# Gated linear attention ahead of two dense layers: units of 128 tokens computed as two halves of 64

## What is computed

```python
f = 1.0 / (1.0 + np.exp(-f_logit))
for t in range(S):
    state = f[:, :, t, :, None] * state + np.einsum('bhd,bhe->bhde', k[:, :, t], v[:, :, t])
    y[:, :, t] = np.einsum('bhd,bhde->bhe', q[:, :, t], state)
x = y.transpose(0, 2, 1, 3).reshape(B * S, H * D)
h = x @ w_in                                   # first block
x = (np.maximum(h, 0) + np.log1p(np.exp(-np.abs(h)))) @ w_out
h = x @ w2_in                                  # second block
out = np.where(h >= 1, h, np.where(h <= -1, 0, (h + 1) ** 2 / 4)) @ w2_out
```

## Time and profile before

| | |
|---|---|
| median of 3 runs | 919.57 us (918.11 to 922.22) |
| the profiled execution: its own time, and its span | 920.22 us, 918.3 us |
| TensorE matmul, weight load | 898.0 us (98%), 742.0 us (81%) |
| VectorE, ScalarE, GpSimd | 512.9 us, 446.4 us, 67.3 us |
| granted TensorE clock over the span | 0.998 of 2.4 GHz |

### The profile page before, as it was taken

One profiled execution on the slowest core, in us unless ns is written; L12 is line 12 of the kernel. 1 busy time (PEld: TensorE's weight loads), 2 busy tenths in 40 slices (PEclk: granted clock), 3 DMA queues, 4 the chain that ended last, 5 costly groups with the idle time before them and its releaser, 6 DMA issues.

```text
span 918.3 us, 14986 instructions
## 1 busy us (share of the span) xinstructions
PE 898.0 (98%) x5810; PEld 742.0 (81%) x5810; DVE 512.9 (56%) x875; ACT 446.4 (49%) x839; POOL 67.3 (7%) x59
## 2 busy tenths in 40 slices
PE   7889999999999999999999999999999999999996
PEld 4789988888888888888888888888888888888884
DVE  5976765566555555654355655555555555555453
ACT  5876665565565555665577533232332332333222
POOL 2112211111111111110000100000000000000000
PEclk9999999999999999999999999999999999999999
DMA  8622222112111311400033200200200200200001
GB/s 276 208 80 65 84 70 74 43 42 77 43 42 54 96 55 42 149 33 1 23 116 98 75 1 1 69 1 1 70 1 0 69 1 1 70 1 10 25 1 37
DMA packets 22300, 50.57 MB, mean 55 GB/s; under 512 B 2384, under 2 KB 3152, under 8 KB 22224
## 3 DMA queue, kind: packets, MB, share of 16 engines
q1 hardware_dynamic: 22224, 49.55, 17.2%
HBM read 40.11 MB, written 9.44 MB: 54 GB/s over the span
## 4 chain that ended last, share of the span: by engine, by line
PE 92%; DVE 2%; ACT 2%; issue 1%; DMA 1%; POOL 1%; SPq 0%; DVEq 0%
PE h_ps L458 15%; PE h_ps L460 14%; PE h_ps L459 14%; PE y_ps L458 14%; PE y_ps L460 14%; PE y_ps L459 14%; PE a_ps L514 2%; PE c_ps L528 1%; PE a_ps L557 1%; PE c_ps L540 1%; PE c_ps L547 1%; PE c_ps L532 1%; PE c_ps L502 1%; DMA qkf_sb<-qkf 1%; POOL qkf_sb L433 1%
## 5 line engine op out<-in xcount | busy, mean ns | idle before, releaser
L818 DVE TENSOR_TENSOR g_lo<-gate,g_hi 128x512 fp32r<-128x512 f32 (+1 forms) x208 | 135.2, 650 | 355.3 <-ACT g_hi L664 354.4
L458 PE MATMUL h_ps<-x_hi,w_hi 128*128 128x512 f32 (+1 forms) x624 | 237.9, 381 | 4.4 <-issue 2.1
L458 PE MATMUL y_ps<-g_hi,w_hi 128*128 128x512 f32 (+1 forms) x624 | 233.4, 374 | 3.5 <-DVE g_lo L818 3.5
L459 PE MATMUL h_ps<-x_lo,w_hi 128*128 128x512 f32 (+1 forms) x624 | 232.8, 373 | 0.0
L460 PE MATMUL h_ps<-x_hi,w_lo 128*128 128x512 f32 (+1 forms) x624 | 232.7, 373 | 0.0
L460 PE MATMUL y_ps<-g_hi,w_lo 128*128 128x512 f32 (+1 forms) x624 | 232.6, 373 | 0.0
L459 PE MATMUL y_ps<-g_lo,w_hi 128*128 128x512 f32 (+1 forms) x624 | 232.5, 373 | 0.0
L652 ACT ACTIVATE soft<-h_ps 128x512 f32<-128x512 f32 x96 | 57.4, 598 | 266.1 <-PE h_ps L460 265.0
L648 ACT ACTIVATE soft<-h_ps 128x512 f32<-128x512 f32 (+1 forms) x112 | 60.0, 536 | 169.7 <-PE h_ps L460 169.7
L458 PEld LDWEIGHTS h_ps<-x_hi,w_hi 128*128 128x128 f32 x624 | 117.3, 188 | 29.4 <-issue 4.7
L458 PEld LDWEIGHTS y_ps<-g_hi,w_hi 128*128 128x128 f32 x624 | 117.4, 188 | 25.9 <-DVE g_lo L818 5.3
(11 more groups left out here) (76 smaller groups left out, 619.1 us busy)
## 6 DMA issues: line engine op xcount, KB each, us to landing
w_raw<-w SPq DMA_DIRECT2D x32, 384.0 KB, 6.0
qkf_sb<-qkf SPq DMA_DIRECT2D x24, 448.0 KB, 4.5
v_sb<-v SPq DMA_DIRECT2D x24, 256.0 KB, 4.5
qkf_sb<-qkf SPq DMA_DIRECT2D x24, 224.0 KB, 3.0
qkf_sb<-x_mid SPq DMA_DIRECT2D x6, 768.0 KB, 5.5
out<-y_sb SPq DMA_DIRECT2D x18, 256.0 KB, 2.2
x_mid<-y_sb SPq DMA_DIRECT2D x15, 256.0 KB, 2.3
x_mid<-y_sb SPq DMA_DIRECT2D x6, 128.0 KB, 1.9
```

The source lines that it names most:

```text
L458: nc.tensor.matmul(out_ap, hi1, hi2, start=start, stop=False, skip_group_check=True)
L459: nc.tensor.matmul(out_ap, hi1, lo2, start=False, stop=False, skip_group_check=True)
L818: nc.vector.tensor_tensor(g_lo[:, t % 2, 0:g.n], gate[:, t % 2, 0:g.n], g_hi[:, t % 2, 0:g.n].bitcast(F32), ALU.subtract).then_inc(glo_don ...
```

## The change

Units of 4 and later are computed as two halves of 64 tokens. Scores are then taken only within a half (four blocks of 64 by 64 for each pair of heads, on four quarters of the array), and half 1 gets what half 0 added through an extra state `mid`. The result of half 0 goes to bank `c_ps`, that of half 1 to `b_ps`. In `result` the part from scores uses row tile 0 for half 0 and row tile 1 for half 1. The part from states puts the even heads on row tile 0 and the odd ones on row tile 1, first each into the bank that its row tile has used so far and then, after a wait of TensorE for its own matmuls (`own_done`), into the other bank. `increment` of a unit moves behind `turn_keys` and in front of `score` of the next unit, and `result` of a unit comes one slot after that. The main slots of units 4 to 23 are 4 slots of the program earlier in full groups, those of units 4 to 8 all fall into the second group of two (slots 1, 4, 7, 10 and 12 of it), and stages of an empty unit 24 end the chain.

```diff
-MAIN = {2: (7, 12), 3: (3, 7, 11), 4: (0, 4, 8, 12)}
+HALVES = (0, 1, 1, 2, 3)
+HALVES_FAST = (0, 1, 1, 2, 3)
+FAST_STEPS = (1, 4, 7, 10, 12)
...
+def make_steps():
+    out = {2: 7, 3: 12}
+    for u in range(B, UNITS + 1):
+        out[u] = FT + FAST_STEPS[u - B] if u <= 2 * B else 2 * FT + 4 * (u - 2 * B - 1)
...
SP:
                         if u < UNITS:
+                            sp.wait_ge(e_done, u - RING + 1)
+                            load_f(u)
                             unit_left(u - RING)
-                            load_unit(u)
+                            load_qk(u)
+                            load_v(u)
...
GpSimd:
+            pool.memset(state[:], 0.0).then_inc(consts, 1)
+            pool.memset(mid[:], 0.0).then_inc(consts, 1)
...
TensorE:
+            def increment(u):
+                pe.wait_ge(k_tok_done, u + 1)
+                ...
+                for p in range(PAIRS):
+                    for a in range(2):
+                        for half, bank in ((0, a_ps), (1, b_ps)) if has_future(u) else ((0, a_ps),):
+                            t = slice(half * T2, (half + 1) * T2)
+                            mm = nc.tensor.matmul(bank[64 * a:64 * a + D, 5 * T2 + p * D:5 * T2 + (p + 1) * D],
+                                                  k_tok[t, p, 64 * a:64 * a + D], vu[t, 2 * p + a, data_columns(a)], ...)
+            def score(u):
+                pe.wait_ge(q_done, u + 1)
+                for p in range(PAIRS):
+                    for half in range(2):
+                        for a, bank in ((0, a_ps), (64, b_ps)):
+                            mm = nc.tensor.matmul(bank[t, (p + 1) * T2:(p + 2) * T2], k[a:a + D, p, t], q[a:a + D, p, t], ...)
+            def result(u):
+                pe.wait_ge(masked, masks_until(min(u + 1, UNITS - 1)))
+                pe.wait_ge(k_tok_done, min(u + 2, UNITS))
+                pe.wait_ge(total_done, states_until(u) - B)
+                for a in range(2):
+                    for k, columns in ((2 * a, main_columns(a)), (1, rest_columns(a))):
+                        for j in range(PAIRS):
+                            for half, t in enumerate(tokens):
+                                nc.tensor.matmul(result_ps(half, k)[HALF * j:HALF * (j + 1), :], vu[t, 2 * j + a, columns],
+                                                 sc[t, a, j, :], ...)
+                pe.wait_ge(state_done, u - B + 1)
+                pe.wait_ge(mid_done, u - B + 1)
+                for other in range(2):
+                    for main in (True, False):
+                        for j in range(PAIRS):
+                            for a in range(2):
+                                half = a ^ other
+                                ... mm = nc.tensor.matmul(result_ps(half, ...), st[rows, first:first + HALF], q[rows, j, tokens[half]], ...)
+                    if other == 0:
+                        mm.then_inc(own_done, 1)
+                        pe.wait_ge(own_done, u - B + 1)
...
+                    if s == 0:
+                        pe.wait_ge(xlo_done, max(u - 1, B))
+                        turn_keys(u); increment(u - 1); score(u)
+                    if s == 2:
+                        result(u - 1)
...
VectorE (mask at stage 1 of unit u, middle(u - 1) behind it; the state at stage 4):
+            def mask(u):                      # one instruction for both banks, 128x1024
+            def middle(u):
+                nc.vector.tensor_tensor(block(mid), increment_ps(a_ps), block(state[:, batch(u)]), ALU.add)
+                nc.vector.tensor_tensor(total[0:ROWS], increment_ps(b_ps), block(mid), ALU.add)
+        # stage 4: state = total * by, by = a 112x4 copy made in prep_end
```

More of the change, by code:

```diff
@@ L166, in build @@
         k_tok = sb("k_tok", [P, PAIRS, ROWS])
-        state = sb("state", [P, B, PAIRS, HEAD])
+        state = sb("state", [P, B, PAIRS * HEAD + REST])
+        mid = sb("mid", [P, PAIRS * HEAD + REST])
+        total = sb("total", [P, PAIRS, D])
+        by = sb("by", [P, B, PAIRS])
         causal = sb("causal", [P, P])
+        causal2 = sb("causal2", [P, T2])
         ident = sb("ident", [P, P])
@@ L272, in same_banks_before, with place, half_scores, block @@
             return 0 if u == 2 else u - 1
+        def place(u):
+            g = [g for g in LAYER0 if g.unit <= u][-1]
+            return g, slice((u - g.unit) * P, (u - g.unit + 1) * P)
+        def half_scores(u):
+            return scores[:, u % 2].rearrange("p b t -> p (b t)").rearrange("p (a b t) -> p a b t", a=2, b=PAIRS)
+        def block(t):
+            return t[0:ROWS, 0:PAIRS * HEAD].rearrange("p (q e) -> p q e", q=PAIRS)[:, :, REST:HEAD]
+        def increment_ps(bank, first=5 * T2):
+            return bank[0:ROWS, first:first + PAIRS * D].rearrange("p (q e) -> p q e", q=PAIRS)
+        def result_ps(half, k):
+            return (c_ps, b_ps)[half][:, k * T2:(k + 1) * T2]
+        def both_halves():
+            return att_ps[:].rearrange("p (n c) -> p n c", n=3)[:, 0:3:2, 0:KT * T2].rearrange("p n (k t) -> p n k t", k=KT)
+        def by_half(x):
+            return x.rearrange("p k (n t) -> p n k t", n=2)
         def first_splits(slot):
@@ L452, in _ @@
             split_w(2 * FT - 1)
-        @block.tensor
+        @engines.tensor
         def _(pe):
@@ L516, in score, with result_whole @@
                 mm.then_inc(sc_done, 1)
-            def result(u):
-                c_ps, q, sc = banks(u)[2], qkf_sb[:, u % RING, 0], scores_of(u)
+            def result_whole(u):
+                c_ps, sc, vu = banks(u)[2], scores_of(u), v_sb[:, u % RING].rearrange("p (h e) -> p h e", h=H)
                 pe.wait_ge(k_tok_done, u + 1)
[L521 to L533, removed]
@@ L534, in result @@
                 pe.wait_ge(v_in[u % RING], 16 * (u // RING + 1))
                 pe.wait_ge(masked, 2 * u + 2)
[L536 to L542, removed]
@@ L543, in result @@
-                t = slice(2 * P, 3 * P)
-                for a in range(2):
[L545 to L548, removed]
+                for a in range(2):
+                    for j in range(PAIRS):
+                        nc.tensor.matmul(c_ps[HALF * j:HALF * (j + 1), 2 * a * P:(2 * a + 1) * P], vu[:, 2 * j + a, main_columns(a)],
+                                         sc[:, a, j, :], start=(a == 0), stop=True, skip_group_check=True)
@@ new lines, in main @@
+            def main(u, s):
+                if whole(u):
+                    if s == 0:
+                        main_whole(u)
+                    if s == 1:
+                        result_whole(u)
+                        increment_whole(u)
+                else:
+                    if s == 0:
+                        pe.wait_ge(xlo_done, max(u - 1, B))
+                        if u < UNITS:
+                            turn_keys(u)
+                        if not whole(u - 1):
+                            increment(u - 1)
+                        if u < UNITS:
+                            score(u)
+                    if s == 2 and not whole(u - 1):
+                        result(u - 1)
@@ L578, in body @@
                     down(g, slot - 2)
-                    for u, s in main_at(g, slot, EARLY_STAGES_PE):
+                    for u, s in main_at(g, slot, WHOLE_PE):
                         main(u, s)
@@ L877, in main, with decay, main_whole @@
             def main(u, s):
-                j = u % RING
+                if whole(u):
+                    main_whole(u, s)
+                    return
+                if s == 1:
+                    if u < UNITS:
+                        mask(u)
+                    if u > B:
+                        middle(u - 1)
+                if s == 4 and u > B:
+                    split_halves(u - 1)
+                    if has_future(u - 1):
+                        dve.wait_ge(total_done, u - B)
+                        dve.wait_ge(ya_done, u)
+                        nc.vector.tensor_tensor(block(state[:, batch(u - 1)]), total[0:ROWS], decay(u - 1),
+                                                ALU.mult).then_inc(state_done, 1)
+            def decay(u):
+                return by[0:ROWS, batch(u), :, None].to_broadcast([ROWS, PAIRS, D])
+            def main_whole(u, s):
                 a_ps, b_ps, c_ps = banks(u)
@@ L904, in split_x, with split_halves @@
+            def split_halves(u):
+                g, c = place(u)
                 dve.wait_ge(xhi_done, u + 1)
```

232 lines of the change are left out of this document (143 added, 89 removed).

## The result

The changed kernel takes 912.58 us (median of 9 runs, 910.49 to 915.62). The kernel before took 919.66 us in the 9 runs beside it, and the ratio is 0.9921, with a 95% interval from 0.9901 to 0.994. That is a gain of 7.1 us where 14.5 were forecast. The sign and the range held; the size was wrong by half.

The account below looks back on a forecast made before the run. TensorE's matmuls, covering 98% of the span, were taken as the bound. Terms -12.8 (third to fifth groups), -2.9 (sixth), +0.3 (second), 0 (first), +0.9 (start) sum to -14.5 us: 905.7 us profiled, median 905.1, range 898 to 924.

Parts of the forecast that it names:

- TensorE's busy time bounds the kernel; eight tiles run together: Whole kernel: TensorE's matmuls cover 98% of the span; sets of eight small tiles take 0.058 us each.
- The main rival: Small matmuls: eight tiles don't hold; 912 to 924 us if partly or by four (0.13), towards 973 (0.06); chance 0.19.
- Stage 0, 1.60 us: Per unit on TensorE: transposes, increment of the unit before, scores and shape changes sum to 1.60 us.
- Own wait, 0.32: Middle of each result: TensorE waits for its own last matmul, 0.32 us, range 0.12 to 0.45.
- Sixteen sets at 0.058 us in the result, 0.93 us: Each result: 128 records for scores and states, eight at a time, take 0.93 us, before 1.54.
- the third to fifth groups: Four units each, every unit gaining 1.07 us: 12 x 1.07 = -12.8 us.
- the sixth: Sixth group: unit work falls from 14.9 to 12.0 us, -2.9 us.
- refill 0 to 0.15: Each result: refilling an emptied queue and four more waits ahead of it cost 0.05 us, between 0 and 0.15.
- Second group, +0.3 us: Second group: -3.1 us of work, +3.4 us of waits for the queries (2.2) and for `total` and `mid` (1.2).
- the second rival: Second group and full groups: late VectorE or loads make TensorE wait, 9 us more, 914; chance 0.15, 909 to 916.
- Start, +0.9 us: Kernel start: clearing `state` and `mid` ahead of `ident` and the two `by` copies cost 0.9 us, 0.3 to 2.
- First group, 0: First group: VectorE and the weights lead there, so no change, from -0.5 to +1 us.

Follow-up runs that it names:

- the long stream: Changed kernel with the score matmuls of each result of units 4 to 23 issued a second time, with all 64 moving columns: 941.59 us, one run.
- both edits: Changed kernel with x_lo split one slot earlier in the second group and GpSimd's keys of unit 8 behind the queries of unit 7: 907.59 us, ratio 0.9857.
- the clears moved too: Those two edits of the changed kernel, plus the memsets of state and mid moved behind ident, TensorE waiting for six constants: 907.05 us, ratio 0.9862.
- the edit for `x_lo`: Changed kernel with x_lo of a unit split one slot earlier on VectorE in the second group: 910.25 us, ratio 0.9891.
- the edit for GpSimd: Changed kernel with GpSimd multiplying the keys of unit 8 after the queries of unit 7 instead of before: 910.93 us, ratio 0.991.
- unit 4 moved: The 907.05 us kernel with unit 4's main slot moved from slot 1 to slot 0 of the second group: 908.56 us, ratio 0.9888.
- all moved: Changed kernel with x_lo one slot earlier in the second group and main slots of units 4 to 7 one slot earlier: 911.49 us, ratio 0.9907.
- the second own wait: Changed kernel with one more wait of TensorE for its own last matmul, between scores and states of each result: 920.0 us, one run.
- the 32-column copies: Changed kernel with the score matmuls of each result of units 4 to 23 issued a second time, with 32 moving columns: 940.48 us, one run.

## Why the prediction was right in sign and wrong in size

- *TensorE's busy time bounds the kernel; eight tiles run together.* Right. The main rival (no more than four, or a floor for every record) fell: 0.0077 us a record in the second half of the states, 0.0098 in the long stream. The floor of about 25 ns between starts that the Trainium skill states ("TensorE: Matmul & The Clock Gate", section "Wait — 56ns, not 53.3ns?") doesn't hold across tiles: the measured distances are under half of it.
- *Stage 0, 1.60 us.* 1.57.
- *Own wait, 0.32.* A hole of 0.30 between starts in the timeline, 0.25 for an added one.
- *Sixteen sets at 0.058 us in the result, 0.93 us.* Mis-sized. The set of eight was right as long as matmuls were at hand; the parts measured 0.66 + 0.30 + 0.24 = 1.20 us, 0.27 more, with 0.05 set aside for the refill. A result is 1.84, not 1.62, and a unit gains 0.88 by the timelines (0.85 by the stretches), not 1.07: 0.2 x 12 = 2.4 us in the third to fifth groups, and in the sixth a good part of the 1.2 us that it fell short (2.9 forecast, 1.7 measured). The prediction's bound, "refill 0 to 0.15", took one emptying of the queue and not the pace behind it.
- *Second group, +0.3 us.* This step failed, by 7.9 us. The two waits that it priced came smaller than forecast (queries 1.2 for 2.2, `total` 0.3 for 1.2). It left out the wait of the turned keys for `x_lo`, 3.2 us, although the diff shows both the wait and the slots 3 and 2 apart (1.1 us of it is the long scan, which no row of the kernel before shows); it left out ScalarE's `y_sb` and VectorE's `g_lo`, 1.4; and it left out that standing has a second price. The clock was at half for 3.4 and 3.5 us, half of which is lost, another 3.4 us in the profiled execution. With the 0.2 us more for each of four results (0.9) these are 3.2 + 1.4 + 3.4 + 0.9 - 1.0 - 0.9 = 7.0 of the 7.9; of the rest some 0.6 us is standing that the list of waits doesn't count (6.7 in the stretch for 6.1 in the list), and the remainder is not traced.
- *VectorE or a load in front of TensorE*, the second rival, had the right mechanism and nearly the time (914), but in another place: it looked at `total` and at full groups, where no wait showed. The misses lay in the group with slots of 2.2 us. That its 914 came near the 912.58 is luck: it priced waits in the full groups, which never came.
- *Start, +0.9 us.* The first dense matmul is 0.3 later (0.4 by the edges of the stretches), inside the forecast's bounds, but by another way. The fills do start 1.2 us later, as the prediction said; the time doesn't pass on, since the load of the first keys sets the start.
- *First group, 0.* 0.9 us shorter. Some 0.5 of it is the shorter hole at its end (1.5 us for 2.1): in the kernel before an `inv` of 0.68 us stood ahead of the `x_lo` that ends it.
- The last matmul starts 4.3 us earlier than before, the span ends 6.9 us earlier. The stores at the very end thus took 2.6 us less; the other kernels of this study lie between. It was not looked into, and stays open.

The forecast's span was 905.7 - 1.9 = 903.8 us, the measured one is 911.4, 7.6 more. Of these 7.9 are the second group and 3.8 the full groups and the sixth; the first group (0.9), the start (0.5) and the end (2.6) give 4.0 back; that is 7.7, the rest is rounding.

## What to carry to other kernels

When slots of a schedule are drawn together, go through every semaphore of the moved step, not only those that look new, and set the slot in which it is signalled against the slot in which it is awaited; the one overlooked here has a slack of one slot where main slots are 4 apart and none where they are 3 apart. Remember that a hole on TensorE may cost clock as well: in the profiled executions half of the 6.6 us that two small edits won in the second group was clock. Don't count low stretches from one profile, since their number changes from execution to execution. Look at how VectorE's operations lie to those of GpSimd: here a scan of 0.4 us took 1.5. A "hole by issue" can be read from the program: look for what the next instruction waits for there. A long run of small float32 matmuls is priced by the matmul, not by its columns.

The best version here is the changed kernel with both edits, 907.59 us (907.05 with the clears moved too): 1.4% under the kernel before by the ratios, and 0.6% under the changed one.

## What the runs showed of the hardware

- *Pace of small matmuls.* Eight tiles of 32 columns run together and 64-column matmuls start 0.007 us apart, but a sustained stream of float32 ones gives one every 0.017 to 0.020 us, at 32 moving columns as at 64.
- *The clock.* TensorE's granted clock fell to 1.2 GHz for 3.4 us at a time, once for 6.9. Wherever it fell in a second group, a hole of 1.4 us or more between two starts had ended at most 1.8 us before, or was still open: holes of 1.4 us (ending at 107.42) and 2.0 (at 117.67) in the changed kernel, 2.2 (at 107.57) with the edit for `x_lo`, 2.0 (at 114.81) with the edit for GpSimd, 2.6 (at 69.32) with unit 4 moved; with all moved it began inside the hole of 4.0 us. Such a hole alone doesn't bring a fall: there was none behind one of 1.8 us (at 94.92) in the changed kernel, one of 2.3 at the group's start in the kernel before, one of 2.0 (at 120.88) with the second own wait, nor in the whole second group with the 32-column copies, with holes up to 2.2 us. Nor is it the same in every execution of one kernel: the changed one's nine have spans from 908.5 us, at a mean clock of 1.000, over 911.4 at 0.996 to 913.7 at 0.994.
- *VectorE beside GpSimd.* A scan of 112 x 128 takes VectorE 0.40 to 0.43 us, and 1.51 to 1.54 when it starts 0.03 to 0.04 us behind a multiplication on GpSimd, in 30 cases of 30.
- *Instruction loads.* With 64 more matmul records in each result, TensorE stood for 1.3 to 2.3 us in about every third result (a list of six or seven holes for 20 results), beside loads of instructions, as told above. The changed kernel, with its 17 packets more than before, shows no such hole.
